# Weighting three batches' tokens for the slots inside the last MLP, and two more early places for expert weights

## The chip, the cores and the metric

One Trainium2 chip, one core. The metric is the device time of one execution in microseconds (us). Three runs of the kernel before took 764.19, 765.50 and 765.57 us, median 765.5 us. The profile is of a further execution, of 765.94 us.

## The reference, cut to what matters

Three stages follow each other: attention (4 batches, 8 heads, 576 tokens, 64 wide), a dense MLP, and a soft mixture of experts. Only the last is touched by the change. `x` is the MLP's output, 2304 tokens of 512.

```python
logits = x @ phi                          # 2304 x 32 slots
d = np.exp(logits - logits.max(0))        # over the tokens, a column for each slot
d /= d.sum(0) + 1e-09
slot_input = (d.T @ x).reshape(8, 4, 512) # 8 experts, 4 slots each
h = np.maximum(slot_input[e] @ w1[e], 0)  # w1[e] is 512 x 1024
slot_out[e] = h @ w2[e]                   # w2[e] is 1024 x 512
c = softmax(logits, over the slots)
return c @ slot_out                       # 2304 x 512
```

The maximum and the sum in `d` run over all 2304 tokens, so that no token has its final weight before the last batch's logits are there.

## The kernel before, in words

The attention of a batch runs with the MLP of the batch before it. The last batch's MLP (m = 3) runs alone. An MLP is 64 units, numbered u = 0 to 63: four quarters of 16, of which eight units (kind 0) make hidden values and eight (kind 1) add to the output `x2t`. A unit is twelve matmuls of 288 columns (L1204), in one of two PSUM banks. For kind 0, ScalarE makes a tanh (`gate`, L736), VectorE the hidden value (`hid`, L925), ScalarE and GpSimd its high and low parts (`gh`, `gl`); for kind 1 VectorE adds to `x2t` (L930, L932). MLP weights come in pieces of 256 KB to two places of `stage` by the SP queue (L497); ScalarE (L675) and GpSimd (L660) split each in two parts, and PE waits for all four pieces of a group of eight units.

The order of the work is written out by hand. `last_units` and `mlp_steps` (L97 to L128) give one list of steps for the last MLP, and **every engine walks through this same list in its own stream**, doing its own part of each step. A step of VectorE stands behind its part of the unit before it, which waits for that unit's matmuls.

A finished batch leaves 5 tiles of tokens in `x2tok`, its logits in `logits` and its maxima in `gm`. Steps `logits`, `token` and `turn` in the next MLP do this for batches 0 to 2. For the last batch, step `post 0` (ahead of unit 62) does tiles 0 and 1, and step `post 1`, after unit 63, tiles 2 to 4: logits (`slot_logits`, L1142), and transposes of the tokens (`turn_last`, L1154), the last tile's behind the next step.

Then the tail begins: VectorE copies the logits (`keep_turned`), PE turns them (L1148), VectorE takes the batch's maxima (L884), all maxima (`gmax`, L943); PE turns these (L1217), VectorE reduces to a maximum for each slot (L945) and a diagonal (L947), PE spreads it (L1221), VectorE subtracts it from all 20 tiles of logits (L950), ScalarE takes the exponential (L754), and 20 matmuls (two passes each, 40 instructions, L1232) weight the 20 tiles of tokens for the slots, four at a time in four column groups of the array. VectorE divides by the sum (L964 to L968), eight matmul instructions add up the column groups and turn the result (L1243), VectorE copies it to `slot_t` (L973). `busy` (L1159) issues matmuls whose result nobody reads, between these steps.

Then come 8 experts: `up` (L1256), ReLU (L761), transposes (L1282), `down` (L1295), and beside them the split and transposes of the combine weights (L1267); at the end 20 matmuls (L1312) and the output's copies and stores.

Expert weights are 16 matrices of 2 MB. They go in order to a ring of NR = 10 places: `ring_a` (4), `ring_b` (5), `ring_x` (1). The first four are loaded in the last MLP, a half (1 MB) at each u with j = 2; places 4 to 8 as `post 1` on the SP queue; place 9 (`ring_x`, in the memory of `x2tok`) when the weighting has ended; matrices 10 to 15 as the experts free places. All by L505.

Of the kernel before, what the change touches and what calls it, by code (L numbers as in the profile page):

```python
# [22 lines left out]
F32 = mybir.dt.float32  # L23
# [41 lines left out]
LAST_POST = ((0, 1), (2, 3, 4))  # L65
RING = 4
# [3 lines left out]
BUSY = (9, 3, 14)  # L70
# [53 lines left out]
def last_units():  # L124

    m = BATCH - 1
    return (held_steps(m) + mlp_steps(m, 0, U_MLP - 2) + [(0, ("post", 0))]
            + mlp_steps(m, U_MLP - 2, U_MLP) + [(0, ("post", 1))])  # L128
# [104 lines left out]
def build(nc, q, k, v, f, w_in, w_out, phi, w1, w2, out):  # L233
    ctx = ExitStack()
    with ctx:
# [17 lines left out]
        x2tok = sb("x2tok", [P, 3 * QT, MODEL], F32, x2_mem)  # L253
        x2_mem.close()

        ring_x = sb("ring_x", [P, 4096])
        ct4 = sb("ct4", [P, BATCH * QT, P], F32R)
        c4 = sb("c4", [P, QT, 4, SLOTS], F32R)
        sb("x2_rest", [P, 3 * QT * MODEL - 4096 - BATCH * QT * P - QT * 4 * SLOTS])
        logits = sb("logits", [P, BATCH * QT, SLOTS])  # L260
# [3 lines left out]
        gm = sb("gm", [P, BATCH, SLOTS])  # L264
# [52 lines left out]
        x2last = sb("x2last", [P, QT, MODEL], F32, tail_a)  # L317
        ring_a = [sb(f"ring_a{i}", [P, 4096], F32, tail_a)[:, :] for i in range(4)]
        ew = sb("ew", [P, BATCH * QT, SLOTS], F32, tail_a)
# [6 lines left out]
        gmax = sb("gmax", [P, SLOTS], F32, tail_b)  # L326
        smax = sb("smax", [SLOTS, 1], F32, tail_b)
        dmax = sb("dmax", [SLOTS, SLOTS], F32, tail_b)
        sel4 = sb("sel4", [P, SLOTS], F32, tail_b)
        bmax = sb("bmax", [P, SLOTS], F32, tail_b)  # L330
        es4 = sb("es4", [P, 4, SLOTS], F32, tail_b)
        den = sb("den", [P, 1], F32, tail_b)
        rden = sb("rden", [P, 1], F32, tail_b)
        part = sb("part", [P, MODEL], F32, tail_b)
        slot_t = sb("slot_t", [P, KM, SLOTS], F32, tail_b)
        ox = sb("ox", [P, P], F32, tail_b)
        so4 = sb("so4", [P, MODEL], F32R, tail_b)
        tail_b.close()
        NOUT = BATCH * QT

        room = x2last[:, :, :].rearrange("p i n -> p (i n)")
        hx = room[:, 0:512].rearrange("p (e n) -> p e n", e=2)
        hxt = room[:, 512:1024].rearrange("p (e c n) -> p e c n", e=2, c=2)
        so_t = room[:, 1024:1536].rearrange("p (t r s) -> p t r s", t=KM, r=4)

# [987 lines left out]
```

## Time and profile before

| | before |
|---|---|
| median of 3 runs | 765.5 us (764.19 to 765.57) |
| profiled execution | 765.94 us, of which the span of the instructions is 764.2 us |
| busy share of TensorE (PE) / its weight loads (PEld) | 94% / 89% |
| busy share of VectorE (DVE) / ScalarE (ACT) / GpSimd (POOL) | 58% / 57% / 52% |
| mean granted TensorE clock | 0.983 of 2.4 GHz |
| last matmul of unit 63 ends, experts begin, last instruction | 686.6, 702.6, 764.2 us |

Times of rows count from the span's start. A row of the timeline gives the start, the duration, the engine, the line, what is written and read, and in brackets how long the engine had been idle and who ended that. PEclk is the granted clock as a share of 2.4 GHz; 0.50 is 1.2 GHz. A duration of a matmul includes its way through the array; between back-to-back matmuls the starts tell the cost. An engine's idle time costs something only where the chain of waits runs over that engine.

### The profile page before, as it was taken

Reading aid. Unit: us, or ns where it says so; the run is one execution under the profiler, and the core shown is the slowest. Engines: PE = TensorE matmul, PEld = TensorE weight load, DVE = VectorE, ACT = ScalarE, POOL = GpSimd, SP = SyncE. Lnnn points to the kernel's source line nnn. Section 1 sums busy time; section 2 is a strip of 40 time slices with the busy share of each in tenths; the row PEclk is TensorE's granted clock in tenths of the full one; section 3 lists DMA queues with packets and bytes.
Section 4 is the critical chain, followed back from the end, with each engine's and each line's share of the span. In section 5 each row is a group of like instructions: output and inputs, shape, how many; then the busy total and the mean of one; then the engine's idle time right before and its main releaser. Section 6 shows DMA issues by size and latency. Waiting matters only on the chain.

```text
span 764.2 us, 15776 instructions
## 1 busy us (share of the span) xinstructions
PE 717.7 (94%) x6027; PEld 681.0 (89%) x6027; DVE 444.7 (58%) x1255; ACT 437.0 (57%) x1031; POOL 399.3 (52%) x439
## 2 busy tenths in 40 slices
PE   3999979999999999999999999999999999998993
PEld 3888879999999999999999989999999999995562
DVE  5898957676776646675656466766542332224323
ACT  4788866575757675666576665757554344311113
POOL 4355357474747764565657564848385476520000
PEclk9999989999999999999999999999999999998897
DMA  4433323332333333333331413332214454598976
GB/s 104 106 92 106 94 65 89 87 94 81 95 94 96 95 94 81 87 105 91 100 91 51 126 28 95 94 108 67 69 43 141 135 169 163 161 401 348 357 307 247
DMA packets 90362, 96.65 MB, mean 126 GB/s; under 512 B 61296, under 2 KB 61296, under 8 KB 88240
## 3 DMA queue, kind: packets, MB, share of 16 engines
q1 hardware_dynamic: 90288, 95.66, 40.6%
q8 instruction: 48, 0.79, 0.4%
q14 instruction: 26, 0.21, 0.1%
HBM read 90.84 MB, written 4.79 MB: 125 GB/s over the span
## 4 chain that ended last, share of the span: by engine, by line
PE 79%; DVE 10%; ACT 7%; issue 2%; DMA 0%; POOL 0%; SPq 0%; DVEq 0%; POOLq 0%
PE mb L1204 51%; PE yb L1057 6%; PE zb L1076 6%; PE xb L1103 5%; PE mb L1256 2%; DVE prob L838 2%; PE xb L1037 2%; ACT prob L689 2%; PE yb L1295 1%; ACT xh L713 1%; DVE ptl L844 1%; PE yb L1059 1%; DVE kl L806 1%; DVE qs L802 1%; ACT qs L681 1%
## 5 line engine op out<-in xcount | busy, mean ns | idle before, releaser
L1204 PE MATMUL mb<-xh,wih 128*128 128x288 f32 x512 | 159.1, 311 | 7.8 <-DVE xl L855 4.3
L1204 PE MATMUL mb<-gh,woh 128*128 128x288 f32 x512 | 156.5, 306 | 3.5 <-DVE x2t L932 3.5
L1204 PE MATMUL mb<-xl,wih 128*128 128x288 f32 x512 | 151.6, 296 | 0.0
L1204 PE MATMUL mb<-xh,wil 128*128 128x288 f32 x512 | 151.6, 296 | 0.0
L1204 PE MATMUL mb<-gl,woh 128*128 128x288 f32 x512 | 150.8, 294 | 0.0
L1204 PE MATMUL mb<-gh,wol 128*128 128x288 f32 x512 | 150.8, 294 | 0.0
L643 POOL TENSOR_TENSOR gl<-hid,gh 128x288 fp32r<-128x288 f32 x128 | 105.0, 825 | 74.9 <-ACT gh L730 73.3
L925 DVE SCALAR_TENSOR_TENSOR hid<-gate,mb 128x288 f32<-128x288 f32 x128 | 57.7, 451 | 116.0 <-ACT gate L736 114.9
L689 ACT ACTIVATE prob<-prob,m_row 64x576 f32<-64x576 f32 (+4 forms) x160 | 96.4, 604 | 35.3 <-DVE m_row L824 34.4
L660 POOL TENSOR_TENSOR wol<-stage,woh 128x512 fp32r<-128x512 f32 x64 | 82.9, 1295 | 62.0 <-ACT woh L675 62.0
L660 POOL TENSOR_TENSOR wil<-stage,wih 128x512 fp32r<-128x512 f32 x64 | 82.1, 1290 | 57.0 <-ACT wih L675 56.9
L1204 PEld LDWEIGHTS mb<-xh,wih 128*128 128x128 f32 x512 | 97.2, 190 | 11.4 <-DVE hid L925 5.9
L1204 PEld LDWEIGHTS mb<-gh,woh 128*128 128x128 f32 x512 | 96.3, 188 | 4.4 <-DVE x2t L932 4.4
L736 ACT ACTIVATE gate<-mb 128x288 f32<-128x288 f32 x128 | 52.5, 410 | 80.6 <-PE mb L1204 80.1
L1204 PEld LDWEIGHTS mb<-xl,wih 128*128 128x128 f32 x512 | 97.2, 190 | 0.0
L1204 PEld LDWEIGHTS mb<-xh,wil 128*128 128x128 f32 x512 | 96.9, 189 | 0.0
L1204 PEld LDWEIGHTS mb<-gl,woh 128*128 128x128 f32 x512 | 96.3, 188 | 0.0
L1204 PEld LDWEIGHTS mb<-gh,wol 128*128 128x128 f32 x512 | 96.0, 188 | 0.0
L824 DVE CUSTOM_DVE_ANT_0 prob<-yb,cum_b 64x576 f32<-64x576 f32 (+4 forms) x160 | 83.6, 537 | 11.4 <-issue 10.8
L702 ACT CAST pth<-zb 128x512 fp32r<-128x512 f32 (+1 forms) x128 | 62.7, 490 | 46.3 <-PE zb L1076 45.1
L932 DVE SCALAR_TENSOR_TENSOR x2t<-mb,x2t 128x288 f32<-128x288 f32 x96 | 43.4, 455 | 71.5 <-PE mb L1204 71.3
L844 DVE TENSOR_TENSOR ptl<-zb,pth 128x512 fp32r<-128x512 f32 (+1 forms) x128 | 73.1, 571 | 17.4 <-ACT pth L702 16.6
(196 smaller groups left out, 1471.1 us busy)
## 6 DMA issues: line engine op xcount, KB each, us to landing
stage<-in_moe_w_in SPq DMA_DIRECT2D x64, 256.0 KB, 3.0
stage<-in_moe_w_out SPq DMA_DIRECT2D x64, 256.0 KB, 2.6
ring_a<-in_moe_w SPq DMA_DIRECT2D x16, 1024.0 KB, 6.9
ring_b<-in_moe_w SPq DMA_DIRECT2D x14, 1024.0 KB, 11.8
cum_b<-cum_dram SPq DMA_DIRECT2D x32, 288.0 KB, 3.7
qk_in<-in_q SPq DMA_DIRECT2D x32, 144.0 KB, 3.0
qk_in<-in_k SPq DMA_DIRECT2D x32, 144.0 KB, 3.5
v_in<-in_v SPq DMA_DIRECT2D x32, 128.0 KB, 3.2
```

The lines of the kernel that those rows point to most:

```text
L643: pool.tensor_tensor(gl[:, i % FT, HALF * (i // FT):HALF * (i // FT + 1)], hid[:, i % RING, :], gh[:, i % FT, HALF * (i // FT):HALF * (i / ...
L660: pool.tensor_tensor(lo[:, t, :], stage[:, t % 2, :], hi[:, t, :].bitcast(F32), ALU.subtract).then_inc(w_lo, 1)
L689: nc.scalar.activation(prob[0:r, par, POFF[i]:POFF[i] + w], prob[0:r, par, POFF[i]:POFF[i] + w], ACT.Exp, bias=m_row[0:r, par, i:i + 1], s ...
L702: nc.scalar.copy(pth[:, lo:hi], zb[:, c % 2, 0:hi - lo]).then_inc(p_hi, 1)
L736: nc.scalar.activation(gate[:, j % RING, :], bank_of("unit", m, u)[:, 0:HALF], ACT.Tanh, scale=GATE / 2).then_inc(h_tanh, 1)
L824: nc.vector.tensor_tensor_reduce(prob[0:r, par, o:o + w], ybf[0:r, base:base + w], cum_b[0:r, par, 0:w], 1.0, 3e38, ALU.add, ALU.min, m_ro ...
L844: nc.vector.tensor_tensor(ptl[:, lo:hi], zb[:, c % 2, 0:hi - lo], pth[:, lo:hi].bitcast(F32), ALU.subtract).then_inc(p_lo, 1)
L925: nc.vector.scalar_tensor_tensor(out=hid[:, j % RING, :], in0=gate[:, j % RING, :], scalar=1.0, in1=bank[:, 0:HALF], op0=ALU.add, op1=ALU. ...
L932: nc.vector.scalar_tensor_tensor(out=dst, in0=bank[:, 0:HALF], scalar=0.5, in1=dst, op0=ALU.mult, op1=ALU.add).then_inc(unit_out, 1)
L1057: mm(ybf[:, base + k0:base + k0 + kw], qs[:, par, P * i:P * i + P], x[:, par, k0:k0 + kw], start=not last, stop=last, skip_group_check=True)
L1076: ins = tr(zb[:, c % 2, at:at + P], prob[:, par, POFF[i] + P * kt:POFF[i] + P * kt + P], swapped if back else ident)
L1204: ins = mm(bank[:, 0:HALF], a[:, t, P * (j % 4):P * (j % 4) + P], x[:, t, cols], start=(i == 0), stop=(i == 11))
```

## The change

Batches 0 to 2 are weighted inside the last MLP, against their own maximum, in new steps of the common list: `top` after unit 22, `spread` after 24, `weigh` after 26, four steps of matmuls after 30 to 33, `keep` after 34, which leaves the sum of 15 tiles in an accumulator `acc` in SBUF. After the MLP only the last batch's 5 tiles are weighted, against the larger of the two maxima of each slot; the accumulator is scaled by `kept` (a factor for each slot), and another factor brings the four column groups to one maximum. Of the last tiles' transposes, the first two of four are done in a step between units 62 and 63, and three quarters of their logits before unit 63's output is read. The batch's own logits for the combine are turned later, beside this. `ring_x` has two places, loaded after units 38 to 52; ring places 0 to 3 are loaded in quarters (512 KB) at odd u below 32. NR = 11, and `ring_x` now comes before `ring_b`.

```diff
-BUSY = (9, 3, 14)
+BUSY = (2, 3, 3)
+EARLY = 3 * QT
+EARLY_AT = {"top": 22, "spread": 24, "weigh": 26, "send0": 30, "send1": 31, "send2": 32, "send3": 33, "keep": 34}
+RING_X_AT = 38
 # mlp_steps
+        if m == BATCH - 1:
+            steps += [(0, ("early", kind)) for kind in EARLY_AT if EARLY_AT[kind] == u]
 # last_units
-            + mlp_steps(m, U_MLP - 2, U_MLP) + [(0, ("post", 1))])
+    ... + [(0, ("post", 0))] + mlp_steps(m, U_MLP - 2, U_MLP - 1)
+            + [(0, ("post", 1))] + mlp_steps(m, U_MLP - 1, U_MLP) + [(0, ("post", 2))])
-        ring = ring_a + ring_b + [ring_x[:, :]]
+        ring = ring_a + ring_x + ring_b
 # SP, unit u of the last MLP
-                    if last and j == 2:
+                    if last and u % 2 and u // 8 < len(ring_a):
                         sp.wait_ge(x_lo, 4 * BATCH)
-                        load_half_expert(u // 16, u % 16 // 8)
+                        load_expert_part(u // 8, u // 2 % 4, 4)
+                    at = u - RING_X_AT
+                    if last and at >= 0 and at % 2 == 0 and at // 8 < len(ring_x):
+                        sp.wait_ge(acc_made, 1)
+                        load_expert_part(len(ring_a) + at // 8, at // 2 % 4, 4)
 # ACT
+                elif st == ("early", "weigh"):
+                    act.wait_ge(ew_sub, 1)
+                    nc.scalar.activation(ew[:, :, :], ew[:, :, :], ACT.Exp).then_inc(ew_exp, 1)
...
+                elif st == ("post", 2):
+                    act.wait_ge(max_made, 2)
+                    nc.scalar.activation(et, last_logits[:, 0:P + 64], ACT.Exp, bias=low_max[:, 1:2], accum_out=bsum)
+                    nc.scalar.activation(kept, low_max[:, 0:1], ACT.Exp, scale=-1.0, bias=low_max[:, 1:2])
+                    ... # copy of tile 2's second half
+            act.wait_ge(top_spread, 1)
+            nc.scalar.activation(factor, top_back[:, 0:1], ACT.Exp, bias=top[:, 0:1]).then_inc(factor_made, 1)
+            nc.scalar.copy(x2last[:, 3, P * AHEAD:MODEL], last_tokens[3][:, P * AHEAD:MODEL]).then_inc(token_out, 1)
 # DVE
+                elif st == ("post", 0):
+                    nc.vector.memset(last_logits[32:64, P:P + 64], -3e38)
+                    nc.vector.memset(last_logits[64:P, P:P + 64], -3e38).then_inc(edge_made, 1)
+                elif st == ("post", 2):
+                    dve.wait_ge(post_logits, m + 2)
+                    nc.vector.tensor_reduce(bmax, last_logits[:, 0:P + 64], AX_X, ALU.max)
+                    nc.vector.tensor_scalar(low_max[:, 1:2], bmax, -1.0, low_max[:, 0:1], ALU.mult, ALU.min)
+            def early(kind):
+                if kind == "top":
+                    for i in range(4):
+                        at = ident[32 * i:32 * i + 32, 32 * i:32 * i + 32]
+                        nc.vector.tensor_copy(sel4[32 * i:32 * i + 32, :], at)
+                        ins = nc.vector.tensor_copy(blk4[32 * i:32 * i + 32, :, :],
+                                                    at.unsqueeze(1).broadcast_to([32, 4, SLOTS]))
+                    ins.then_inc(sel_made, 1)
+                    dve.wait_ge(l_kept, 2 * BATCH - 2)
+                    nc.vector.tensor_reduce(gmax, gm[:, 0:BATCH - 1, :], AX_X, ALU.max).then_inc(gmax_made, 1)
+                elif kind == "spread":
+                    dve.wait_ge(gmax_turned, 1)
+                    nc.vector.tensor_reduce(smax, top_row[0:SLOTS, 0:P], AX_X, ALU.max)
+                    nc.vector.tensor_scalar(dmax, ident[0:SLOTS, 0:SLOTS], smax[:, 0:1], None, ALU.mult)
+                elif kind == "weigh":
+                    ... # subtract the maxima from 15 tiles of logits
+                elif kind == "send0":
+                    ... # sums of the weights
+                elif kind == "keep":
+                    dve.wait_ge(early_sent, 1)
+                    nc.vector.tensor_copy(acc[:, :], early_sent_ps).then_inc(acc_made, 1)
 # DVE, after the last MLP
+            ... # top, half of tile 4, row_s, row, two copies to ewt, all_sum, part_sum
+            dve.wait_ge(den_made, 1)
+            ... # den, rden, sel_f
+            dve.wait_ge(sent, 1)
+            nc.vector.scalar_tensor_tensor(out=acc, in0=acc, scalar=kept, in1=last_sent, op0=ALU.mult, op1=ALU.add)
+            dve.wait_ge(slots_summed, 1)
+            nc.vector.tensor_copy(slot_t, slot_ps)
 # PE
+                elif st == ("post", 0):
+                    pe.wait_ge(edge_made, 1)
+                    pe.wait_ge(acc_made, 1)
+            def early(kind):
+                if kind == "top":
+                    pe.wait_ge(gmax_made, 1)
+                    tr(top_row[0:SLOTS, 0:P], gmax[:, :], ident[:, :]).then_inc(gmax_turned, 1)
+                elif kind == "spread":
+                    pe.wait_ge(dmax_made, 1)
+                    mm(top_back[:, 0:SLOTS], ones[0:SLOTS, :], dmax[:, :], start=True, stop=True)
+                    mm(top_back[:, SLOTS:SLOTS + 1], blk4[0:SLOTS, :, :], smax[:, :], start=True, stop=True)
+                elif kind == "keep":
+                    mm(top_row[:, 0:1], es4[:, :, :], ones[:, 0:1], start=True, stop=True)
+                elif kind != "weigh":
+                    pe.wait_ge(ew_exp, 1)
+                    for t in range(first, min(first + 4, EARLY)):
+                        ins = mm(early_sent_ps[32 * g:32 * g + SLOTS, :], ew[:, t, :], x2tok[:, t, :], ...)
 # PE, after the last MLP
+            tr(top_row[0:1, 0:P], low_max[:, 1:2], ident[:, :]).then_inc(top_turned, 1)
+            busy(BUSY[0], last_sent)
+            turn_slots(last_turn, et).then_inc(e_turned, 1)
+            mm(top_back[:, 0:1], row, ident[0:1, 0:1], start=True, stop=True).then_inc(top_spread, 1)
+            busy(BUSY[1], last_sent)
+            pe.wait_ge(ewt_made, 1)
+            pe.wait_ge(token_out, 1 + QT * BATCH)
+            ... # 5 matmuls for the last batch's tiles, sent
+            mm(top_row[:, 0:1], blk4, part_sum, start=True, stop=True).then_inc(den_made, 1)
+            turn_slots(last_turn_l, lt).then_inc(lt_last_turned, 1)
+            busy(BUSY[2], top_back)
+            pe.wait_ge(acc_made, 2)
+            ... # 4 matmuls of acc with sel_f
+            def turn_slots(bank, x):
+                tr(bank[:, 0:P], x[:, 0:P], ident[:, :])
+                return tr(bank[0:64, P:P + SLOTS], x[0:SLOTS, P:P + 64], ident[0:SLOTS, 0:SLOTS])
```

## Rows read from the trace of the kernel before

**Rows 1.** Stretches by windows: length, busy us and instructions by engine, clock, DMA share, GB/s.

```profile
640.00:686.00 46.00, 46.00 (x358) 45.64 (x357) 12.77 (x28) 16.63 (x39) 24.12 (x25) 1.00 0.70 257
711.30:745.00 33.70, 32.85 (x741) 22.14 (x729) 10.39 (x34) 4.25 (x14) 0.00 (x0) 1.00 0.82 334
```

**Rows 2.** Chain of waits, end of the MLP to the experts: start, us, what.

```profile
683.40 3.20 PE mb L1204 x24
...
687.14 1.07 PE yb L1142 x16
688.20 1.02 PE xb L1154 x8
...
694.11 4.50 PE xb L1232 x40
698.61 0.33 PE zb L1238 x2
...
700.16 2.09 PE xb L1243 x8
702.27 0.30 DVE slot_t L973
702.62 3.64 PE mb L1256 x32
...
707.42 3.53 PE mb L1256 x32
...
713.86 1.84 PE mb L1256 x32
```

**Rows 3.** VectorE in the last MLP around units 22 and 24, by the timeline.

```profile
619.86 0.46 DVE L925 SCALAR_TENSOR_TENSOR hid<-gate,mb 128x288 f32<-128x288 f32 x1 [0.17 <-ACT gate L736]
```

**Rows 4.** ScalarE in the same stretch.

```profile
619.42 0.41 ACT L736 ACTIVATE gate<-mb 128x288 f32<-128x288 f32 x1 [0.87 <-PE mb L1204]
```

**Rows 5.** Groups of instructions by shape, 681 to 703 us: count, busy us, mean ns.

```profile
L955 DVE COPY sel<-ident 32x32 f32<-32x32 f32 x4 | 0.7, 171 | 0.0
...
L943 DVE TENSOR_REDUCE gmax<-gm 128x32 f32<-128x128 f32 x1 | 0.4, 370 | 0.0
...
L888 DVE COPY logits<-l 128x160 f32<-128x160 f32 x1 | 0.2, 232 | 0.0
```

**Rows 6.** VectorE after the MLP, by the timeline.

```profile
686.62 0.46 DVE L932 SCALAR_TENSOR_TENSOR x2t<-mb,x2t 128x288 f32<-128x288 f32 x1 [1.14 <-PE mb L1204]
...
691.26 0.28 DVE L945 TENSOR_REDUCE smax<-zb 32x1 f32<-32x128 f32 x1 [0.38 <-PE zb L1217]
...
699.35 0.75 DVE L968 TENSOR_SCALAR part<-xb,rden 128x512 f32<-128x512 f32 x1
...
700.67 0.17 DVE L971 MEMSET yb<- 128x128 f32 x1
```

**Rows 7.** ScalarE reading 256 columns of PSUM, by the timeline.

```profile
706.28 0.38 ACT L761 ACTIVATE x2last<-mb 128x256 f32<-128x256 f32 x1 [9.66 <-PE mb L1256]
```

**Rows 8.** GpSimd's last split of a group of MLP weights (unit 16).

```profile
605.57 1.29 POOL L660 TENSOR_TENSOR wil<-stage,wih 128x512 fp32r<-128x512 f32 x1 [1.05 <-ACT wih L675]
```

**Rows 9.** TensorE at the begin of unit 16.

```profile
608.10 0.29 PE L1204 MATMUL mb<-xh,wih 128*128 128x288 f32 x1
```

**Rows 10.** DMA issues from 703 us on: count, KB each, median us to landing.

```profile
ring_b<-in_moe_w SPq DMA_DIRECT2D x4, 1024.0 KB, 16.6
```

**Rows 11.** Stretches around changes of the granted clock, columns as in Rows 1.

```profile
97.00:100.30 3.30, 0.21 (x2) 0.00 (x0) 1.34 (x4) 2.43 (x5) 3.30 (x3) 1.00 0.55 125
100.30:107.10 6.80, 5.61 (x24) 5.59 (x25) 2.19 (x3) 2.43 (x6) 1.85 (x3) 0.50 0.00 0
...
251.50:254.00 2.50, 1.14 (x9) 0.91 (x8) 1.49 (x3) 2.31 (x5) 2.50 (x3) 1.00 0.00 0
...
701.00:704.00 3.00, 2.62 (x22) 1.65 (x25) 1.20 (x5) 0.00 (x0) 0.00 (x0) 0.51 1.01 414
...
748.90:752.20 3.30, 3.30 (x9) 2.54 (x8) 2.76 (x4) 2.50 (x5) 0.00 (x0) 0.50 0.65 251
```

More of the change, by code:

```diff
@@ L263, in build @@
         lt = sb("lt", [P, P + 64])
-        gm = sb("gm", [P, BATCH, SLOTS])
+        bmax = sb("bmax", [P, 1])
+        low_max = sb("low_max", [P, 2])
+        kept = sb("kept", [P, 1])
+        bsum = sb("bsum", [P, 1])
+        all_sum = sb("all_sum", [P, 2])
         e5 = sb("e5", [P, QT, SLOTS])
@@ L426, in build @@
         C_CHAIN = 5
-        t_dve = sem("t_dve")
-        t_act = sem("t_act")
-        t_pe = sem("t_pe")
-        sel_made = sem("sel_made")
+        gmax_made = sem("gmax_made")
+        gmax_turned = sem("gmax_turned")
+        smax_made = sem("smax_made")
+        dmax_made = sem("dmax_made")
+        early_spread = sem("early_spread")
+        ew_sub = sem("ew_sub")
+        ew_exp = sem("ew_exp")
+        es_made = sem("es_made")
+        early_sent = sem("early_sent")
+        early_den = sem("early_den")
+        edge_made = sem("edge_made")
+        ahead_out = sem("ahead_out")
+        max_raw = sem("max_raw")
+        max_made = sem("max_made")
+        e_made = sem("e_made")
+        kept_made = sem("kept_made")
+        e_turned = sem("e_turned")
+        ewt_made = sem("ewt_made")
+        sent = sem("sent")
+        acc_made = sem("acc_made")
+        sum_made = sem("sum_made")
+        sel_made = sem("sel_made")
+        top_made = sem("top_made")
+        top_turned = sem("top_turned")
+        row_made = sem("row_made")
+        top_spread = sem("top_spread")
+        factor_made = sem("factor_made")
+        den_in = sem("den_in")
+        den_added = sem("den_added")
+        den_made = sem("den_made")
+        sel_scaled = sem("sel_scaled")
+        slots_summed = sem("slots_summed")
+        slot_made = sem("slot_made")
+        lt_last = sem("lt_last")
+        lt_last_turned = sem("lt_last_turned")
+        result_turned = sem("result_turned")
+        result_hi = sem("result_hi")
+        result_made = sem("result_made")
         up_done = sem("up_done")
@@ L497, in load_w, with load_expert_part @@
                 sp.dma_start(stage[:, slot, :], src).then_inc(w_dma[slot], 16)
-            def load_half_expert(e, half):
+            def load_expert_part(e, part, parts):
                 w = (w1[e // 2].rearrange("(p t) n -> p t n", t=KM) if e % 2 == 0
@@ L503, in load_half_expert @@
                 dst = ring[e % NR].rearrange("p (t n) -> p t n", t=KM)
-                half_of = slice(KM // 2 * half, KM // 2 * (half + 1))
-                sp.dma_start(dst[:, half_of, :], w[:, half_of, :]).then_inc(e_dma[e % NR], 16)
+                some = slice(KM // parts * part, KM // parts * (part + 1))
+                sp.dma_start(dst[:, some, :], w[:, some, :]).then_inc(e_dma[e % NR], 16)
             def load_expert(e):
-                load_half_expert(e, 0)
-                load_half_expert(e, 1)
+                load_expert_part(e, 0, 2)
+                load_expert_part(e, 1, 2)
             def load_qk(b, s):
@@ new lines, in _ @@
+            dve.wait_ge(sent, 1)
+            dve.wait_ge(acc_made, 1)
+            nc.vector.scalar_tensor_tensor(out=acc[:, :], in0=acc[:, :], scalar=kept[:, 0:1], in1=last_sent,
+                                           op0=ALU.mult, op1=ALU.add).then_inc(acc_made, 1)
+            dve.wait_ge(slots_summed, 1)
+            nc.vector.tensor_copy(slot_t[:, :, :], slot_ps[:, 0:KM * SLOTS].rearrange("p (t s) -> p t s", t=KM)).then_inc(slot_made, 1)
+            dve.wait_ge(lt_last_turned, 1)
+            keep_logits(last_turn_l)
@@ L1140, in slot_logits @@
+            def slot_logits(bank, tiles, t0, t1):
+                for t in range(t0, t1):
                     for i in tiles:
@@ L1167, in wait_bank @@
                     pe.wait_ge(o_sum, BATCH * HEADS)
+                    if kind == "turn":
+                        pe.wait_ge(token_out, 1 + QT * m + QT)
                     return
```

333 lines of the change are left out of this document (199 added, 134 removed).

## The prediction

> **What bounds the kernel now.** I read the windows first. In the last MLP, from 640 to 686 us, TensorE is busy for 46.00 of 46.00 us while VectorE works 12.77 and ScalarE 16.63 us; in the experts, from 711.3 to 745 us, it is busy for 32.85 of 33.70 us [rows 1]. So TensorE sets the end in both, and what is put on it, or makes it wait, inside the MLP costs its full time. Between the two lies a hand-over, and the chain of waits shows it: the last matmul of unit 63 ends at 686.60 (683.40 + 3.20) and the experts begin at 702.62, 16.0 us later [rows 2]. Of these the 20 weighting matmuls take 4.50, the sum of the column groups 2.09, and the rest is small instructions of VectorE and ScalarE, one after another. The change shortens this hand-over and pays in the MLP. The question is only which is larger.
>
> **Added to the MLP: 10.6 us.** All engines walk through one list, so the order in a step decides.
>
> *Step `top`, 3.0 us.* PE waits for `gmax_made` right behind unit 22. VectorE makes it in the same step, that is behind its own part of unit 22, which needs unit 22's matmuls and the tanh. Today the tanh of unit 22 starts at 619.42, when its matmuls have just ended [rows 4], and the hidden value is done at 619.86 + 0.46 = 620.32 [rows 3]: 0.92 us in which PE would stand. Then come eight copies. A 32 x 32 copy takes 0.17 us and four take 0.7 [rows 5]; a copy of 128 columns has no row and lies between that 0.17 and the 0.23 of 160 columns [rows 5]; I take 0.20, so 0.7 + 0.8 = 1.5. Then the maxima of 96 values, 0.33 (128 take 0.37 [rows 5]), and hand-overs of some 0.03 each. The hole is 2.9 us, and the transpose behind it 0.13. Nothing covers the hole: PE's queue is in order.
>
> *Step `spread`, 1.75 us.* PE waits for `dmax_made` behind unit 24, and VectorE first does unit 24's output (0.46), then a reduction (0.28) and a small product (0.17 to 0.28) [rows 6]; with hand-overs the hole is 1.1. Two matmuls with 128-column weights follow, at the 0.33 of the sum of the weights today [rows 2].
>
> *The matmuls, 4.2 us.* Twenty tiles take five rounds of four, 4.50 us, so 0.90 a round [rows 2]; fifteen take four rounds, 3.6. They are cut in four and each has a change of shape before and behind it. No row prices that; bounds are 0 and 0.15 a step, and I take 0.07, so 3.9. `keep` adds one matmul, 0.33.
>
> *The end of the MLP, 1.6 us.* `post 0` did not wait; now PE waits there for `edge_made`, which VectorE makes behind unit 61's output: 0.46 and two PSUM memsets, each 0.12 to 0.17 [rows 6], with hand-overs 0.84. The step between units 62 and 63 is six transposes; eight take 1.02 [rows 2], so 0.77. They were behind the MLP before, so they are counted here and are gone there.
>
> 3.0 + 1.75 + 3.9 + 0.33 + 0.84 + 0.77 = 10.6 us; by the bounds 9.8 to 11.5. The other new steps (`weigh`, `send0` on VectorE, the exponential) lie several units ahead of their reader and beside idle time, and cost nothing.
>
> **The queues.** On SP the quarters stand ahead of the fourth weight piece of a group. The last split before unit 16 ends at 605.57 + 1.29 = 606.86 [rows 8] and PE needs it at 608.10 [rows 9], a slack of 1.24. A quarter is 0.5 MB; at 0.41 MB per us (334 GB/s at a DMA share of 0.82 [rows 1]) it delays the piece by up to 1.2 us. That just fits: 0, at most +0.5. After `top` the holes themselves give slack. The wait for `acc_made` on SP, after unit 38, comes some 6 us after the accumulator is made; nothing stands behind it. The two further ring places take 4 MB, some 10 us of transfer, out of the time after the MLP, more than the hand-over gets shorter. Today the experts' last matrices land 16.6 us after issue [rows 10] and PE still does not wait in the experts. So the transfers neither gain nor cost.
>
> **Taken from the hand-over: 6.2 us.** Counted from the last matmul of unit 63, the new chain is: nine of the twelve logits' matmuls beside unit 63's output and three behind it, 1.07 [rows 2], no longer a wait of 0.55 ahead of them. Maximum of 192 values 0.35 (128 take 0.28 [rows 6]), its combination 0.17: at 1.75. ScalarE's exponential 0.4 (256 columns take 0.38 [rows 7]), its turn on PE 0.25: at 2.5. VectorE, which has meanwhile copied half of tile 4, makes the row of maxima (0.28, 0.2) and then two copies of the weights: at 3.25. ScalarE makes `kept`, half of tile 2, the factor (which waits for that row and a matmul) and half of tile 3: at 3.75, and this is last. Five matmuls are two rounds, 1.8: at 5.6. The sum's matmul 0.33, three small VectorE operations of 0.2, then the scaled accumulator, 512 columns, at the 0.75 of today's division [rows 6]: at 7.3. The sum of the column groups as today, 2.09, and the copy to `slot_t`, 0.30 [rows 2]: the experts begin at **9.8** instead of 16.0. Bounds are 9.0 (small operations overlap) and 11.6 (the five matmuls at half clock).
>
> **The clock.** The granted clock falls to 0.50 after TensorE was nearly idle: 0.21 busy of 3.30 us from 97 us on, then 0.50 for 6.8 us [rows 11]. It did not fall where 1.14 of 2.50 us were busy [rows 11]. In the hand-over it fell after a gap from 698.94 to 700.16 and the sum of the column groups, whose matmuls have 32 columns [rows 2], and stayed through the first two `up`, 3.64 and 3.53 us instead of 1.84 [rows 2, 11]. The new hole at unit 22 is 2.9 us long, nearer to the 3.1 us without work at 97 than to the 1.36 at 251.5. I take a fall, for one stretch of 3.4 us as at 748.9 [rows 11], which costs half of it, **1.7 us**; between 0 and 3.4 (a stretch of 6.8, which the hole of `spread` could make of it). In the hand-over 5.6 to 9.8 us hold only waits and small matmuls again, so I expect the same fall and the same slow first experts: 0, between −4.0 (both `up` at full clock save 3.5, the transposes between them some 0.5) and +1.
>
> The Trainium skill has a rule against the 1.7: in TensorE: Matmul & The Clock Gate, section "HAM oscillation — how this bites in real kernels", the clock is halved by waits of a kind longer than this hole. By it the MLP would lose nothing here and the result would be that of the second rival. The row at 698.94 speaks against it: a gap of 1.24 us, with little work behind it, was enough.
>
> **Sum.** 10.6 − 6.2 + 1.7 = +6.1 us. On the profiled execution's 765.94 that is 772.0; that execution lies 0.4 above the median of the runs, 765.5, so the forecast for the median is **771.6 us**.
>
> **Rivals.**
> *No fall of the clock in the MLP.* For it: the 1.36 us gap at 251.5 did nothing, and the hole may be split. Against it: it is twice as long. Then 765.5 + 10.6 − 6.2 = 769.9. Chance 0.22.
> *The clock holds in the hand-over.* This is the way to a faster kernel. Its place is the sum of the column groups and the first two `up`. TensorE idles there in three pieces of 0.4 to 0.8 instead of one of 1.24. Its price is −4.0. With the fall in the MLP the result is 767.6, without it 765.9. It makes the kernel faster only when the other terms are under +2.5: with the additions at 9.8, the hand-over at 9.0 and no fall at unit 22 it is 765.5 + 9.8 − 7.0 − 4.0 = 764.3, and with `top`'s copies partly beside each other 763. Against it: the work from 5.6 to 9.8 is as thin as today's. Chance 0.22, of which 0.1 is faster, 0.06 within what can be told, 0.06 slower.
> *The holes of the steps are longer or the clock stays down over two stretches.* 773 to 775.5. Chance 0.1.
> *The early steps do not make PE wait* (the list would have to be ahead on VectorE). Then only 6.6 us of work are added, and with no fall 765.9, no difference. The list speaks against it. Chance 0.04.
> The forecast itself has 0.42.
>
> **Chances.** A measurement of this kernel can tell 0.2%, 1.5 us. Faster by more 0.10, within 0.12 (the parts named, and 0.02 of the first rival's low side), slower 0.78. Range 765.0 to 775.5.
>
> **What would show it.** In the changed kernel's last MLP, PE has a gap of 2.9 us ahead of a transpose `zb<-gmax`, ended by VectorE's `gmax`; one of 1.1 ahead of `zb<-dmax`; one of 0.8 ahead of the logits after unit 61; and four groups of `ew` matmuls of 0.9 us. The clock shows 0.50 for 3.4 us behind the first gap. From the end of unit 63 to the first `up` are 9.8 us, and the first `up` takes some 3.6. The experts are otherwise unchanged, without a wait for a DMA. The forecast is wrong if the first gap is under 1 us, or if the stretch from 9.8 is under 9 or over 11.6, or if both `up` run in 1.84.

## The result and the profile after

Measured in turns on one chip, the kernel after took 777.01 us (median of 4 runs, 773.79 to 778.09), the kernel before 765.54 (4 runs, 764.19 to 766.06): a ratio of 1.0146 [1.0113, 1.0178], 11.5 us slower. The forecast was 771.6, its range 765.0 to 775.5. The sign was right. The size was not: the result lies 1.5 us above the range. Three of the four executions took 777.0 to 778.1 us at a mean granted clock of 0.981 to 0.983, the fourth 773.8 us at 0.988, so part of the size goes with the clock. The profiled execution of after took 777.03 us, its span 775.2, so between the two profiles 775.2 − 764.2 = 11.0 us are to be found. They lie here (ends of units from the timeline of TensorE; "forecast" is the difference that the prediction's terms give; "mixing" is the 20 matmuls at the end, with the output's copies and stores):

| stretch | before | after | difference | forecast |
|---|---|---|---|---|
| MLP, end of unit 0 to 15 | 27.92 | 28.12 | +0.2 | 0 |
| units 16 to 22 | 11.12 | 12.00 | +0.9 | 0 |
| units 23 to 26, with `top` and `spread` | 6.34 | 16.02 | +9.7 | 3.0 + 1.75 + 1.7 |
| units 27 to 34, with the four sends | 12.72 | 17.48 | +4.8 | 3.9 |
| units 35 to 61 | 42.93 | 43.15 | +0.2 | 0.33 |
| units 62 and 63 | 5.21 | 6.91 | +1.7 | 0.84 + 0.77 |
| end of unit 63 to the first `up` | 16.03 | 10.12 | −5.9 | −6.2 |
| experts, to the first mixing matmul | 45.50 | 43.86 | −1.6 | 0 |
| mixing, to the last instruction | 16.04 | 17.24 | +1.2 | 0 |

Where TensorE only computes, next to nothing has changed. Two windows of after, which answer to [rows 1] (busy us and instructions by engine, clock, DMA share, GB/s):

```profile
655.00:695.00 40.00, 40.00 (x304) 40.00 (x303) 11.93 (x26) 15.64 (x37) 24.13 (x25) 1.00 0.68 225
720.00:755.00 35.00, 33.72 (x757) 22.76 (x745) 11.46 (x39) 4.60 (x15) 0.00 (x0) 1.00 0.73 296
```

40.00 of 40.00 us, and then 33.72 of 35.00. The loss is in the holes. The chain of waits of after, from the late weight piece to the second hole (start, us, what):

```profile
600.69 6.24 DMA stage<-in_moe_w_in
...
606.96 0.63 ACT wih L746
...
607.65 1.29 POOL wil L731
...
609.08 3.41 PE mb L1384 x24
...
615.42 4.33 DMA stage<-in_moe_w_out
...
619.77 0.02 ACT woh L746
...
620.29 0.41 ACT gate L823
...
620.73 0.45 DVE hid L1057
...
622.28 0.32 DVE sel L974
...
624.22 0.28 DVE gmax L979
...
624.54 0.28 PE zb L1294
```

What this costs is in the timeline of TensorE (start, us, engine, line, what, and the idle time before it): unit 22's last matmul ends at 620.14 + 0.29 = 620.43, and the next instruction starts at 624.54.

```profile
609.08 0.37 PE L1384 MATMUL mb<-xh,wih 128*128 128x288 f32 x1 [0.65 <-POOL wil L731]
...
620.14 0.29 PE L1384 MATMUL mb<-xh,wil 128*128 128x288 f32 x1
624.54 0.28 PE L1294 MATMUL zb<-ident,gmax 128*32 128x128 f32 x1 [4.11 <-DVE gmax L979]
...
630.94 0.40 PE L1298 MATMUL zb<-dmax,ones 32*128 32x32 f32 x2 [1.42 <-DVE dmax L985]
```

So TensorE stands at `top` and at `spread`, 4.11 and 1.42 us (forecast 2.9 and 1.1), and once where nothing was forecast, 0.65 ahead of unit 16. At the edge, after unit 61, it stands 0.97 (forecast 0.84). What VectorE does in the long hole, by its timeline:

```profile
620.73 0.45 DVE L1057 SCALAR_TENSOR_TENSOR hid<-gate,mb 128x288 f32<-128x288 f32 x1 [2.46 <-ACT gate L823]
621.10 0.82 DVE L1044 TENSOR_TENSOR cw<-e,r 128x160 f32<-128x160 f32 x1
621.84 0.44 DVE L1057 SCALAR_TENSOR_TENSOR hid<-gate,mb 128x288 f32<-128x288 f32 x1
622.20 0.40 DVE L974 COPY sel<-ident 32x32 f32<-32x32 f32 x1
...
622.74 0.67 DVE L974 COPY sel<-ident 32x32 f32<-32x32 f32 x1
...
623.56 0.17 DVE L974 COPY sel<-ident 32x32 f32<-32x32 f32 x1
...
630.24 0.65 DVE L985 TENSOR_SCALAR dmax<-ident,smax 32x32 f32<-32x32 f32 x1
```

and GpSimd's beside it:

```profile
621.69 1.69 POOL L714 TENSOR_TENSOR gl<-hid,gh 128x288 fp32r<-128x288 f32 x2
...
629.60 2.49 POOL L731 TENSOR_TENSOR wil<-stage,wih 128x512 fp32r<-128x512 f32 x2
```

The same copy takes 0.67 us while GpSimd works (until 623.38) and 0.17 when it does not. It ends at 622.74 + 0.67 = 623.41, 0.03 behind GpSimd's instruction; `dmax` ends at 630.89, 0.04 behind the first of the two that start at 629.60. The hidden value of unit 22 ends at 622.28, not 0.92 us after its matmuls but 1.85. Behind the holes the clock falls twice (windows of after):

```profile
620.43:624.54 4.11, 0.00 (x2) 0.00 (x1) 3.68 (x12) 1.22 (x4) 2.92 (x3) 1.00 0.67 239
...
625.30:628.70 3.40, 3.40 (x16) 3.40 (x15) 0.45 (x1) 1.23 (x4) 0.63 (x1) 0.50 0.09 35
628.70:632.10 3.40, 1.99 (x14) 1.74 (x14) 1.29 (x3) 0.97 (x2) 3.38 (x4) 1.00 0.03 11
632.10:635.50 3.40, 3.40 (x17) 3.40 (x16) 0.46 (x1) 0.00 (x0) 0.00 (x0) 0.50 0.87 270
```

3.40 us at 1.2 GHz (0.50), 3.40 at 2.4, 3.40 at 1.2 again. At 2.4 GHz a unit's twelve matmuls take 1.59 us, 0.13 each. At 1.2 GHz their starts lie 0.24 us apart (timeline of TensorE):

```profile
626.07 0.44 PE L1384 MATMUL mb<-xh,wil 128*128 128x288 f32 x1
626.31 0.44 PE L1384 MATMUL mb<-xh,wih 128*128 128x288 f32 x1
```

So 3.4 us at half clock, full of such matmuls, cost 3.4 × (1 − 0.1325 / 0.24) = 1.5 us, a little less than half their length. The hand-over, which answers to [rows 2], in the chain of waits:

```profile
697.12 0.47 DVE x2t L1064
...
698.05 1.07 PE yb L1320 x16
...
702.39 1.60 PE mb L1384 x12
703.99 1.04 PE yb L1320 x16
...
705.05 0.37 DVE bmax L963
...
707.82 2.04 PE mb L1406 x10
...
711.70 2.04 PE xb L1418 x8
...
714.11 3.58 PE mb L1434 x32
...
718.66 1.84 PE mb L1434 x32
```

Unit 63 ends at 703.99, `up` begins at 714.11. The five matmuls (L1406) start 3.83 us after unit 63, where 3.75 was forecast. The first `up` takes 3.58 us, the second 1.84: the half clock that held through both before [rows 2, 11] ends after one.

### The profile page after: what moved, and what is told of

Its sections match the earlier page's. It is cut to its first block, busy times and chain, and to the rows that moved or that the text cites. A ratio compares the mean times of both kernels' runs of the same rounds, so it can differ in the third digit from the quotient of the medians.

```text
span 775.2 us, 15796 instructions
## 1 busy us (share of the span) xinstructions
PE 721.0 (93%) x6018; PEld 682.4 (88%) x6018; DVE 446.2 (58%) x1268; ACT 437.4 (56%) x1039; POOL 399.4 (52%) x439
## 4 chain that ended last, share of the span: by engine, by line
PE 76%; DVE 10%; ACT 7%; issue 2%; DMA 2%; POOL 1%; SPq 0%; DVEq 0%; ACTq 0%; POOLq 0%
PE mb L1384 48%; PE yb L1194 6%; PE zb L1213 5%; PE xb L1240 5%; PE mb L1434 2%; PE xb L1174 2%; ACT prob L760 2%; DVE prob L930 2%; DVE ptl L936 1%; ACT xh L784 1%; PE yb L1473 1%; PE yb L1196 1%; DVE kl L898 1%; DVE qs L894 1%; DMA stage<-in_moe_w_in 1%
## 5 line engine op out<-in xcount | busy, mean ns | idle before, releaser
L916 DVE CUSTOM_DVE_ANT_0 prob<-yb,cum_b 64x576 f32<-64x576 f32 (+4 forms) x160 | 83.6, 538 | 11.1 <-issue 10.5
```

The lines of the kernel that those rows point to most:

```text
L916: nc.vector.tensor_tensor_reduce(prob[0:r, par, o:o + w], ybf[0:r, base:base + w], cum_b[0:r, par, 0:w], 1.0, 3e38, ALU.add, ALU.min, m_ro ...
```

## The experiments

Executions of one kernel scatter by 1.5 to 5 us and the chips differ a little (the kernel before had medians of 762.5 to 765.5 on them). So each kernel is compared with the kernel before on its own chip, and a term's size is read from the stretches of one profiled execution, most of which repeat to 0.1 us where nothing stands or waits.

**The eight copies out of `top`.**

```diff
-EARLY_AT = {"top": 22, "spread": 24, ...
+EARLY_AT = {"copies": 14, "top": 22, "maxima": 22, "spread": 24, ...
 # DVE: the eight copies are step "copies", the reduction to gmax is step "maxima"
```

> Only VectorE's eight copies move, from the step behind unit 22 to one behind unit 14; the maxima of the early batches stay behind unit 22. Theory (order: PE stands behind VectorE's part of the same step, and every instruction there counts): the hole ahead of the transpose of gmax falls from 4.1 to about 2.1 us, and with it one of the two slow clock stretches may go (1.7 us): 777.0 minus 2 to 4, 773 to 775. Rival (the copies are the whole matter, slowed by GpSimd's use of the shared port): hole under 1 us and 771 or less. Rival (the hole is absorbed by slack elsewhere): 777.

772.6 us, ratio 1.011 [1.0064, 1.0155]. The hole is 1.93 us instead of 4.11, and yet the clock falls twice (windows):

```profile
619.70:621.70 2.00, 0.11 (x1) 0.00 (x0) 1.72 (x4) 1.19 (x4) 2.00 (x2) 1.00 0.77 280
622.40:625.80 3.40, 3.40 (x17) 3.40 (x16) 0.45 (x1) 1.03 (x3) 0.58 (x2) 0.50 0.63 210
...
629.20:632.60 3.40, 3.40 (x16) 3.40 (x16) 0.46 (x1) 0.00 (x0) 0.19 (x1) 0.50 0.84 271
```

Without the copies, and with the pieces less late, the hole is 2.2 us shorter (forecast for the copies 1.5). What is left is VectorE's own part of unit 22 and the reduction. The first fall comes at 622.4, ahead of the second hole, so here 1.93 us of idle time were enough for the half clock. The second fall comes behind that second hole, of 1.52 us.

**Copies and maxima behind unit 14, the transpose still at 22.**

```diff
+EARLY_AT = {"copies": 14, "maxima": 14, "top": 22, "spread": 24, ...
```

> VectorE's whole part of the step top, copies and maxima, moves behind unit 14; TensorE's transpose stays behind unit 22. Theory (order): the hole of 4.1 us is gone, the first slow clock stretch (1.7) too, and as the second one began 3.4 us later with only the 1.4 us hole of the step spread in it, it goes as well: 777.0 - 4.1 - 3.4 = 769.5. If the small hole alone makes the clock fall: 771.2. Rival (the clock fell for another reason than the hole): 772.9, with slow stretches in the last MLP still there.

771.41 us, 1.010 [1.0068, 1.0131]. Only the hole of `spread` is left, 1.00 us, and the granted clock reads 1.00 through the whole MLP, behind that hole too (windows):

```profile
624.50:625.50 1.00, 0.02 (x1) 0.00 (x0) 0.87 (x3) 0.42 (x2) 1.00 (x3) 1.00 0.89 365
625.50:632.00 6.50, 6.48 (x49) 6.47 (x50) 2.11 (x6) 1.68 (x3) 2.58 (x3) 1.00 0.62 195
```

Units 23 to 26 take 8.67 us instead of 16.02: 4.11 of hole, 0.42 of the shorter second one and 3.1 of clock (two stretches of 1.5) would be 7.6 less, and 7.35 were measured. Against the gain stands a wait that the long hole had hidden: unit 23 starts 0.42 us behind the transpose and not 0.04, at 621.07, because the hidden value of unit 21, which frees its PSUM bank, ends only at 620.56 + 0.46 = 621.02. The total fell short of the 769.5 expected: in this profile the experts had 10.2 us at half clock and took 45.60 us.

**No holes at all.**

```diff
+EARLY_AT = {"copies": 14, "maxima": 14, "top": 22, "diagonal": 24, "spread": 26, "weigh": 28, ...
 # DVE: smax and dmax are step "diagonal"; PE's two matmuls stay in "spread"
```

> As the run before, and VectorE's part of the step spread stays behind unit 24 while TensorE's goes behind unit 26 and the subtraction and exponential behind unit 28. Theory: no hole ahead of either, no slow clock in the MLP: 777.0 - 4.1 - 1.4 - 3.4 = 768.1. Rival (work, not waiting, is what the early steps cost): 773 or more.

769.27 us, 1.007 [1.0045, 1.0094]. TensorE stands nowhere between units 22 and 61 (the 0.21 us that is missing here is ahead of unit 16):

```profile
608.00:645.00 37.00, 36.79 (x270) 32.27 (x269) 14.51 (x39) 13.41 (x31) 20.42 (x20) 1.00 0.61 204
```

The MLP takes 114.54 us, 9.1 less than in the change and still 8.3 more than before. That is what the work itself, the late piece and the edge cost.

**`ring_a` in halves again.**

```diff
-                    if last and u % 2 and u // 8 < len(ring_a):
+                    if last and j == 2:
-                        load_expert_part(u // 8, u // 2 % 4, 4)
+                        load_expert_part(u // 16, u % 16 // 8, 2)
```

> The four ring_a places are loaded in halves of 1 MB at j = 2 of each eight units again, as before the change; the ring_x places stay early. Theory (a quarter put ahead of the fourth weight piece makes it late): the wait of 0.65 us before unit 16 goes, and the tanh of unit 21 no longer waits behind a late piece on ScalarE, so the hole behind unit 22 is 0.5 to 0.7 shorter: 777.0 - 1.1 - 0.6 = 775.3. Rival (the pieces are late by chance of the queue, not by the quarters): 777.

773.26 us, 1.0134 [1.0097, 1.017]. Now the forecast's hole is there, to 0.05 us (timeline of TensorE):

```profile
622.49 0.39 PE L1294 MATMUL zb<-ident,gmax 128*32 128x128 f32 x1 [2.95 <-DVE gmax L979]
628.35 0.40 PE L1298 MATMUL zb<-dmax,ones 32*128 32x32 f32 x2 [1.00 <-DVE dmax L985]
```

Units 16 to 22 take 11.11 us as before (12.00 in the change), and one stretch of 3.4 us at half clock follows. The DMA view of 596 to 624 us says why: the w_in pieces land after 3.5 us (median) here, 4.5 in the change and 3.7 before, the w_out pieces after 2.9, 3.5 and 2.7. The MLP is 3.9 us shorter than the change's. How late the pieces are varies: in the seven other kernels with quarters TensorE waited 0 to 0.21 us ahead of unit 16 and units 16 to 22 took 11.1 to 11.7 us, and the four of them with the whole of `top` in one step had 3.65, 3.96, 4.18 and 4.43 us between unit 22 and the transpose. All four are above the 2.95 and 2.98 of the two kernels with halves.

**The edge's memsets earlier.**

```diff
-                elif st == ("post", 0):    # DVE: the two memsets
+                elif kind == "keep":       # ... behind the copy to acc
```

> The two memsets for the edge of the last logits move from VectorE's part of the step post 0 to its part of the step keep (behind unit 34). Theory (TensorE waited for them behind unit 61): the wait of 0.97 us goes, and TensorE then waits for nothing there; from the end of unit 61 to the end of unit 62 as before the change, 3.6 us instead of 4.65: 1.0 us less. Rival (the wait only moves, because the logits need unit 61's output anyway): no difference.

773.68 us, 1.0125 [1.0105, 1.0145]. Units 62 and 63 take 5.87 instead of 6.91 us: the edge was worth 1.04 (forecast 0.84). The six transposes are the other 0.66. The rest by which this time is below the change's is not the edge's: in this profile the first hole was 3.65 us and one stretch at half clock followed, not two.

**All fifteen early matmuls in one step.**

```diff
-"send0": 30, "send1": 31, "send2": 32, "send3": 33
+"send0": 30, "send1": 30, "send2": 30, "send3": 30
```

> The fifteen early weighting matmuls are issued in one step behind unit 30 and not in four. Theory (each group costs its 0.9 us and 0.3 us for the change of shape before and behind it, 4.77 in all): 3.6 + 0.3 = 3.9, so 0.9 us less. Rival (the price is in the matmuls, also alone): no difference.

776.02 us, 1.0151 [1.0134, 1.0168]; units 27 to 34 take 16.47 us instead of 17.48. The chain of waits of this kernel:

```profile
637.90 6.77 PE mb L1384 x51
644.67 3.56 PE xb L1310 x30
648.24 6.54 PE mb L1384 x48
```

In one step they are the 3.6 us of the prediction. In four they are 0.99 to 1.00 each, and a unit between two of them takes 1.78 to 1.80 instead of 1.59: a split costs 0.3 us, not the 0.07 that I took nor the 0.15 of the upper bound. The time as a whole does not show it, since this profile's hole at unit 22 was 4.43 us, with 10.2 us at half clock.

**The two `ring_x` places loaded late.**

```diff
-                    if last and at >= 0 and at % 2 == 0 and at // 8 < len(ring_x):
-                        load_expert_part(len(ring_a) + at // 8, at // 2 % 4, 4)
 # behind unit 56 instead, ahead of ring_b's first
+                    for e in (4, 5):
+                        for part in range(4):
+                            load_expert_part(e, part, 4)
```

> The two ring_x places are not loaded behind units 38 to 52 but first of all behind unit 56; all other loads follow. Theory (the two places are what keeps the shorter hand-over free of DMA waits): the last matrix lands 9.8 us later, at 756.5 instead of 746.7 of the changed kernel's own profile, and PE needs it at 753.0: some 3.6 us slower, with a wait of PE for e_dma before the last down. Rival (transfers were never near the path): no difference.

777.76 us, 1.0172 [1.0155, 1.0189], not to be told from the change. The wait that I expected did not come: its last matrices land a median 15.0 to 21.5 us after issue (9.8 and 17.0 in the change), the last at 751.25, the last `down` starts at 752.60, and TensorE waits for none. The early places bring nothing here, as the forecast had it.

**All four repairs.** The diffs of the third, fourth, fifth and sixth experiments together: no holes, halves, the early edge, one step of sends.

> VectorE's parts ahead of TensorE's as in e3_both_early, ring_a in halves as in e4_halves, the memsets early, the early matmuls in one step. Theory: the last MLP is 8.3 - 0.45 - 1.0 - 0.9 = 6.0 us longer than before the change, the hand-over 5.9 shorter, the first experts 1 to 2 shorter by the clock: within 1 us of the kernel before, no difference that can be measured. Rival (the change has a gain that the holes hid): faster by 2 us or more.

766.66 us (12 runs), 1.0025 [1.0013, 1.0036]. TensorE never stands in the MLP, which takes 111.94 us, 5.7 more than before: that is the added work. The hand-over gives 5.9 back. The stretch at half clock in it is as long as before, 10.2 us; the experts take 45.92 us (before 45.50), and the last stretch, from the first mixing matmul, 17.25 (16.04).

**Fills in the hand-over.** The kernel with all four repairs, and matmuls whose result nobody reads between its last steps; then the same fills at the same three places of the kernel before.

```diff
-BUSY = (2, 3, 3)
+BUSY = (2, 3, 8)
             ins.then_inc(slots_summed, 1)
+            busy(2, top_back)
             up(0)
+            busy(3, top_back)
```

> e8_all_four, with matmuls that nobody reads put into TensorE's waits of the hand-over: five more ahead of the sum of the column groups, two behind it, three behind the first up. Theory (the clock falls in the thin stretch of the hand-over, and its slow stretch of 10.2 us costs the first experts 4 us): the granted clock stays at 2.4 GHz there, experts 42 us instead of 45.9, 766.7 - 3.9 = 762.8, faster than the kernel before. Rival (the sum of the column groups itself is too thin, and the clock falls all the same): 766 to 767, with the slow stretch still there but perhaps shorter.

> The kernel before the change, filled in the same three places (eight, two and three matmuls). Theory: the clock stays at 2.4 GHz, experts 41.5 instead of 45.5, 4 us less: 761. Rival: the clock falls all the same, no difference. Also a second look at the stretch from the first mixing matmul to the end, 16.0 us in the one profile of the kernel before, 16.5 to 17.8 in all kernels with the change: if it is 17 here too, it varies by itself; if it is 16.0, it belongs to the change.

With the change: 767.15 us (6 runs), 1.0037 [1.0024, 1.005]. The expected 762.8 was missed: the clock fell all the same, at 701.7 for 6.8 us (two windows):

```profile
700.00:701.70 1.70, 1.52 (x11) 1.41 (x11) 1.03 (x3) 0.00 (x0) 0.00 (x0) 1.00 1.02 410
701.70:708.50 6.80, 6.80 (x48) 3.85 (x49) 1.22 (x5) 0.72 (x2) 0.00 (x0) 0.50 0.81 333
```

In the kernel before they held it at 1.00 where it was 0.50 [rows 11]:

```profile
701.10:711.30 10.20, 10.05 (x171) 6.67 (x175) 2.97 (x11) 1.03 (x3) 0.00 (x0) 1.00 1.00 386
```

and its experts took 42.43 us instead of 45.50. So the forecast's price of the clock in the hand-over, up to 4.0 us, is about right (3.1 measured, with three fills in it). The times do not show it: 763.51 us (12 runs), 0.9993 [0.9982, 1.0005]. The mean granted clock, which is known for every execution, says in part why. Seven of the twelve have the 0.989 of the profiled one (median 762.8 us), the other five 0.982 to 0.987. But the kernel before is better than its profile: its 17 executions on this chip have a median of 0.986, its profile had 0.983. So a typical execution of it has less half clock to win back than the profile shows; where it lies in them is not known.

**Fills in the hole at unit 22.** The change, and its version with halves, with 30 and 20 such matmuls ahead of the wait for `gmax_made`. VectorE's work, and so the start of unit 23, stays. This prices the clock apart from the hole.

```diff
                 if kind == "top":
+                    pe.wait_ge(token_out, 1 + (BATCH - 1) * QT)
+                    busy(30, xb[:, 0, :])
                     pe.wait_ge(gmax_made, 1)
```

> The change, with 30 matmuls whose result nobody reads on TensorE between unit 22 and the wait for the maxima; VectorE's work is as long as before, so the unit after it starts no earlier. It prices the clock apart from the hole. Theory (the first stretch at half clock is an answer to the idle hole, and costs half its length): the fills take about 3.4 us of the 4.1, so the idle time ahead of the maxima's transpose is under 1 us; no stretch at 0.50 near unit 23, perhaps still one of 3.4 us behind the hole at unit 24 (1.0 to 1.4 us, which alone did nothing in the kernel with the top early). Units 22 to 26 take 16.0 - 1.7 = 14.3 us with one stretch gone, 12.6 with both; the time 777.0 - 3.4 = 773.6 us (775.3 with one). Rival (the half clock is no answer to idle time in the hole, but to the change of work, or fills do not count): two stretches as before, 777 us.

> The kernel with ring_a in halves (measured 773.3 us, hole 2.95 us, one stretch of 3.4 us at half clock), and 20 such matmuls in the hole. Theory: the hole is as long for the next unit, idle time under 1 us, no half clock in the MLP; units 22 to 26 take 12.76 - 1.7 = 11.1 us, the time 771.6 us. Beside the kernel with 30 fills it gives the price of the late weight pieces alone, without the clock: theory some 1.5 to 2 us (0.9 of the wait ahead of unit 16 and 0.5 to 1.1 of the longer hole). Rival: the pieces were late only now and then, and the two kernels are within 0.5 us.

With quarters: 774.55 us, 1.0161 [1.0118, 1.0204]. Its timeline of TensorE:

```profile
619.35 3.46 PE L1339 MATMUL xb<-ident_r 128*128 128x128 f32 x30
623.69 0.28 PE L1296 MATMUL zb<-ident,gmax 128*32 128x128 f32 x1 [0.88 <-DVE gmax L979]
```

From unit 22's end (619.51) to the transpose are 4.18 us, nearly as without the fills (4.11), but the granted clock now reads 1.00 from 623.7 to 630, and units 23 to 26 take 12.60 us instead of 16.02. Of these 3.42 us the second hole has 0.42: it is 1.00 us here, as GpSimd does not hold `dmax` up. With the 0.07 by which the first is longer, 3.07 are left for the clock. **The first stretch was an answer to the idle hole, and the two stretches cost 3.1 us**, 1.5 each; that the sum met the 3.4 expected is luck. With halves: 773.57 us, 1.0136 [1.0104, 1.0168], and the timeline of TensorE:

```profile
620.40 2.35 PE L1339 MATMUL xb<-ident_r 128*128 128x128 f32 x20
623.54 0.28 PE L1296 MATMUL zb<-ident,gmax 128*32 128x128 f32 x1 [0.80 <-DVE gmax L979]
```

Units 23 to 26 take 11.41 instead of 12.76 us with a hole as long (2.98 against 2.95), so the one stretch, which began 0.3 us ahead of the transpose, cost 1.4.

The second stretch goes with the second hole. Nine profiled kernels have one: where it was 1.25 to 1.52 us (the change, the copies early, the sends together) a stretch of its own began behind it, where it was 1.0 (six kernels) none did. So in the run with 30 fills the second stretch may be gone by the shorter second hole as well as by the filled first one; no run separates the two.

 Between the two kernels with fills the MLP differs by 1.5 us, the price of the late pieces alone. Their totals are 1.0 us apart and the intervals overlap. Beside the kernels without fills (1.0146 and 1.0134) the ratios show no gain, though the profiles do; that chip's kernel before was itself at 762.5, with runs from 761.2 to 766.3. The profile shows what a term costs in the execution seen, the totals do not resolve it.

## Why the prediction was wrong in size and right in sign

*What bounds the kernel* held. TensorE has no slack in the MLP, so each hole and each added matmul came through, and the hand-over got shorter by about what was worked out. The MLP's terms were forecast at 12.3 us with the clock and came to 17.4. These 5.1 us are the whole miss; the terms behind the MLP were off by +0.3, −1.6 and +1.2 and nearly cancel, which is luck. Of the 5.1 the queues have 2.0, the clock 1.4, the matmuls 0.9, the second hole 0.3, and small terms the rest. What came is the rival with longer holes and two stretches at half clock (773 to 775.5 us, chance 0.1), and more. The prediction's bounds for the added work, 9.8 to 11.5, were narrow and do not follow from its terms, whose own bounds give some 10.1 to 11.1; without the clock 14.4 was measured.

*The queues.* The step that failed first is the sentence that the quarters ahead of the fourth piece "just fit: 0, at most +0.5". The piece took 6.24 us and its split ended at 608.94, not 606.86: 2.1 us later, against a slack of 1.24. TensorE stood idle for 0.65 us, and units 16 to 22 took 0.9 us more. The estimate counted one quarter of 512 KB ahead of the piece at full rate; two more were issued right behind it (601.06), and what each of them cost is not separated. For unit 16 the 0.9 of this profile is a high draw, since the other kernels with quarters had 0 to 0.6. The larger fault is that I priced the delay for unit 16 alone. The w_out pieces were late too (the last landed at 619.74), and there the delay did not end in a wait of TensorE for weights. It went through ScalarE, which casts the piece (L746) ahead of unit 21's tanh, to VectorE, and so into the hole, in every kernel with quarters and `top` in one step. With the halves both are gone (units 16 to 22 at 11.11, hole 2.95). This is 2.1 us of the miss by the profiled execution, 0.9 ahead of unit 22 and 1.2 in the hole; by the pair with fills it is 1.5. TensorE waited for no transfer of expert weights, as forecast.

*Step `top`.* On time the hole is 2.95 us against 2.9 forecast. That is partly luck: in the kernel with halves too one 32 x 32 copy took 0.67 us beside GpSimd, which I had not priced, while the other copies overlapped by some tenths and the maxima took 0.26 instead of 0.33. The rows for the copies came from the tail, where GpSimd is idle (0.00 us busy in the second window of [rows 1]); the step was moved to where it is busy for half the time. That was visible. The Trainium skill, SBUF — State Buffer, section "Who interferes with whom", says that a copy or a tensor-scalar in a two-port mode shares ports with GpSimd and that the one issued second is blocked until the other ends. The trace agrees: 0.67 us against 0.17, and 0.65 against 0.23 for `dmax`, and both end 0.03 to 0.04 us behind GpSimd's instruction.

*Step `spread`.* 1.42 against 1.1 for the hole; 1.00 where GpSimd does not hold `dmax`. The two matmuls take 0.53 us against 0.66, and the transpose of `top` 0.04 against 0.13. But a unit behind a hole takes 1.84 us from its first start to its end (run with 30 fills), where one in the stream adds 1.59; these two times 0.25 were not forecast.

*The clock.* The mechanism was right, the term was mis-sized: 3.1 us instead of 1.7, two stretches at 1.5. I took one stretch as likeliest and named two ("which the hole of `spread` could make of it") as a bound. The change showed two, with a normal stretch between. The run with the top early says that the second hole by itself (1.00 us) does nothing, and the run with the copies early says that 1.93 us followed by 1.52 brings both back. The rival with no fall in the MLP had 0.22 and is refuted by the fills: half clock with 2.95 us of idle time, none with the same hole filled. The rule of the Trainium skill that I had set beside it (TensorE: Matmul & The Clock Gate, "HAM oscillation — how this bites in real kernels") names longer waits than 2.95 us as what halves the clock. The runs with holes of 2.95 and 1.93 us do not agree; the change's own 4.11 us would be long enough for it. (The prediction calls this rival the second; it is the first of its list, at 769.9 us.) All this rests on one profiled execution of each kernel.

*The matmuls.* 4.8 against 3.9: the cost of the four changes of shape, bounded at 0.15 a step and found at 0.3. It lies to two thirds in the unit behind, where I had not looked. *The edge* cost 1.04 against 0.84, the transposes 0.66 against 0.77, `keep` 0.2 against 0.33. The step `turn` ahead of unit 7, whose second transpose got another shape, costs 0.2, unforecast.

*The hand-over.* 10.1 against 9.8. The five matmuls start where forecast (3.83 against 3.75) and take 2.04 instead of 1.8; the rest differs by 0.1.

*The experts.* The same fall of the clock came, as forecast, but it lasted 3.4 us and not 10.2, which gives the 1.6 us. It is not the change's doing: with the same code in the hand-over, the kernels of the experiments show stretches of 3.4, 6.8 and 10.2 us there, and experts of 43.4 to 45.9 us. So the forecast of 0 for the experts is not wrong in kind; what an execution shows there is drawn from this scatter.

*The last stretch.* 1.2 us longer, forecast 0. The kernels with the change took 16.5 to 17.8 us there and the kernel before 16.04, with fills 16.74. The 20 matmuls take 6.5 us in both profiled kernels. The difference lies in the output's stores: the last of them is issued 12.6 and 12.8 us behind the first mixing matmul in the two profiles without the change, and 13.2 to 13.7 in the twelve with it. Why stays open; no run isolates it.

*The sign.* 10.6 us of forecast additions against 6.2 taken away: even without a hole, a late piece or a slow clock the change puts 5.7 us on the bound engine to take 5.9 from the hand-over. So the version with all four repairs is 0.2 us ahead at the begin of `up`, and 1.0025 [1.0013, 1.0036] of the time before at the end: in its profile the experts lose 0.4 us and the last stretch 1.2. No version with the change was faster than the kernel before, and of the fills in the kernel before no gain can be told.

## What to carry to other kernels

When a step is moved from a tail into a stage whose bound engine has no slack, price its instructions with rows from the new place and its neighbours there, not from the old one: the same copy cost four times as much beside GpSimd. A delayed transfer does not only hurt who waits for it; follow it through every engine that handles the piece, since each is in order. And a hole of two microseconds on TensorE cost more than its length here, while the same work made ready a few units earlier cost none of it (9 us between the two orders of the same list).

## What the runs showed that was not expected

- After 4.11 us of idle time the clock went 0.50, 1.00, 0.50 in stretches of 3.4 us each, and after only 1.93 us too; a lone gap of 1.00 us left it at 1.00. Behind the second hole a stretch of its own came at 1.25 to 1.52 us and not at 1.0. Thirty matmuls that nobody reads kept it up and cost nothing, as they stood where TensorE waited.
- Fills of the same number kept the clock up in the hand-over of the kernel before and did not in that of the kernel with the change (6.8 us at 0.50, though TensorE was busy for 1.52 of the 1.70 us ahead of the fall), in the one profiled execution of each.
- Four column groups' matmuls between units of 128 x 128 weights cost 0.1 us in their own step and 0.2 in the unit behind it.
- Beside GpSimd a `cw` product of 160 columns took 0.81 to 1.08 us (alone 0.32), and a 32 x 32 copy up to 1.28 us (alone 0.17).
